# Mixing weights loaded right behind the taps' weight, five mixing and nine output places, another written-out order

## The reference

```python
w = softmax(weight, axis=-1)                       # 8 heads x 7 taps
out = einsum('hk,bskhg->bshg', w, x_unf)           # y: causal convolution of x
wq = y @ w_q; wk = y @ w_k                         # 192 -> 64
W_tok = (1 / sqrt(64)) * einsum('bsd,btd->bst', wq, wk)
mixed = einsum('bst,btd->bsd', W_tok, y)
return maximum(mixed, 0) @ w_out                   # 192 -> 192, float32
```

## Time and profile before

| what | us |
| --- | --- |
| median of three runs | 175.79 (175.0 to 176.97) |
| profiled execution, its own time | 176.94 |
| span of the profiled execution, first to last instruction | 175.2 |
| mean granted TensorE clock, share of full speed | 0.992 |

### The profile page before, as it was taken

How to read it: one execution, slowest core, us unless ns; L and a number is a source line. 1 busy time by engine, 2 the same in 40 slices (tenths; PEclk the granted TensorE clock), 3 DMA queues, 4 the chain that set the end, 5 groups by cost and what they waited for, 6 DMA issues and landing times.

```text
span 175.2 us, 6279 instructions
## 1 busy us (share of the span) xinstructions
PE 146.8 (84%) x2862; PEld 93.4 (53%) x2867; DVE 121.3 (69%) x187; ACT 113.7 (65%) x188; POOL 21.1 (12%) x23
## 2 busy tenths in 40 slices
PE   5987602198899899799999999999999998999980
PEld 1343302184357747465746665677657756675550
DVE  4514300546997799588868786899998859887660
ACT  2331401105993889667899878887988877797950
POOL 7982000200073005000000000000000000000000
PEclk9999999999999999999999999999999999999996
DMA  3999999999959999999920099972068998849796
GB/s 28 174 185 199 193 197 192 192 193 193 178 61 185 194 195 249 225 195 332 384 81 9 4 356 392 382 288 98 4 239 326 388 394 337 345 176 390 298 391 267
DMA packets 45388, 39.88 MB, mean 228 GB/s; under 512 B 35506, under 2 KB 37170, under 8 KB 45362
## 3 DMA queue, kind: packets, MB, share of 16 engines
q0 software_dynamic: 34080, 12.98, 62.5%
q1 hardware_dynamic: 11282, 26.51, 40.3%
HBM read 26.51 MB, written 25.95 MB: 299 GB/s over the span
## 4 chain that ended last, share of the span: by engine, by line
PE 60%; DMA 15%; DVE 9%; SPq 8%; issue 3%; ACT 1%; ACTq 0%; DVEq 0%; POOLq 0%
PE ps L723 12%; PE ps L915 11%; PE ps L898 11%; PE ps L590 10%; SPq L511 7%; DMA whi<-in_moe_w_k_dram 7%; PE ps L655 6%; DMA out_dram<-out_sb 5%; DVE y L622 4%; PE ps L818 4%; DMA xw<-in_x_dram 3%; PE ps L831 2%; DVE out_sb L933 2%; PE ps L278 1%; DVE rt L855 1%
## 5 line engine op out<-in xcount | busy, mean ns | idle before, releaser
L590 PE MATMUL ps<-xw,band 64*64 64x384 bf16 (+4 forms) x480 | 39.3, 332 | 5.8 <-issue 2.0
L723 PE MATMUL ps<-y 128*64 128x192 bf16 (+2 forms) x792 | 29.6, 232 | 12.1 <-ACT y L622 7.8
L933 ACT COPY out_sb<-ps 128x768 f32<-128x768 f32 (+1 forms) x47 | 34.6, 751 | 7.1 <-PE ps L915 6.5
L590 PE MATMUL ps<-xw,carry 64*64 64x384 bf16 (+2 forms) x160 | 38.1, 327 | 0.0
L854 ACT ACTIVATE rt<-ps 128x1024 bf16<-128x1024 f32 (+3 forms) x49 | 34.7, 732 | 4.8 <-PE ps L818 3.6
L622 ACT CAST y<-ps 128x792 bf16<-128x792 f32 (+3 forms) x46 | 30.6, 686 | 10.2 <-PE ps L590 9.8
L622 DVE CAST y<-ps 128x792 bf16<-128x792 f32 (+3 forms) x34 | 27.2, 816 | 13.1 <-PE ps L590 12.8
L723 PEld LDWEIGHTS ps<-y 128*64 128x64 bf16 x792 | 26.7, 118 | 15.5 <-ACT y L622 8.3
L637 DVE STREAM_TRANSPOSE yt<-y 128x768 uint32<-128x768 uint32 x32 | 30.1, 960 | 0.7 <-ACT y L622 0.5
L590 PEld LDWEIGHTS ps<-xw,band 64*64 64x64 bf16 x480 | 17.3, 114 | 21.5 <-PE ps L590 6.1
L855 DVE TENSOR_SCALAR rt<-ps 128x512 bf16<-128x512 f32 (+3 forms) x31 | 23.6, 769 | 7.2 <-PE ps L818 3.5
(11 more groups left out here) (105 smaller groups left out, 107.5 us busy)
## 6 DMA issues: line engine op xcount, KB each, us to landing
out_dram<-out_sb SPq DMA_DIRECT2D x28, 768.0 KB, 6.3
xw<-in_x_dram POOLq DMA_DIRECT2D x7, 816.0 KB, 23.0
xw<-in_x_dram POOLq DMA_DIRECT2D x7, 768.0 KB, 24.9
out_dram<-out_sb SPq DMA_DIRECT2D x8, 384.0 KB, 3.3
xw<-in_x_dram POOLq DMA_DIRECT2D x3, 384.0 KB, 9.0
out_dram<-out_sb SPq DMA_DIRECT2D x8, 96.0 KB, 3.2
xw<-in_x_dram POOLq DMA_DIRECT2D x1, 432.0 KB, 5.6
wq6f<-in_moe_w_q_dram SPq DMA_DIRECT2D x3, 64.0 KB
```

What stands on the lines that cost most here:

```text
L590: lambda p=p, a=a, w=w, back=back: e.matmul(at(op, p, a, z), w, XW[r : r + 64, s, a - back : z - back, g], start=start, stop=not start, sk ...
L723: mm = e.matmul(at[p : p + 64, o : o + z - r], Y[:, yb, c, r : r + 64], Y[:, yb, c, r:z], start=st, stop=end, skip_group_check=True,)
L933: return e.copy(dst, src) if op.letter == "A" else e.tensor_copy(dst, src)
```

## The change

The weight loads no longer wait for the taps' weight and for x; they have to stand behind the taps' weight in SP's order. `RT` has five places instead of four and `OUT` nine instead of ten. `PLAN` is another order of the same 929 operations, with other letters (engines and tilings) and banks in many places. In it SP's order is 0, 51, 49, 52, 50 (k, q, o, t) and then the stores. On ACT the order begins 16, 23, 56 (w_k), 32, 35, 30, 80, 74, 62 (w_out), 68, 71, 86, 101, 92, 61 (w_out), 59 (w_k), 54 (w_q, t), 107, 95, 110, 143, 128, 131, 55 (w_q, t), 113, 122, 116, 152, 53 (w_q). On DVE no cast of a weight other than w_k is left (57, 60, 58).

PE does the same products, of which some change their tiling. Between ACT and DVE some copies change places: ACT has 48 convolution casts (46 before), 42 output copies (47), 32 and 21 of the two relus (25 and 24), 15 scaled copies (8) and 6 of `gsb` (3).

```diff
 PLAN = """
-0S 4D 5D 2D 7D 1D 45G 3D 9D 13F 11G 46G 17D 8D 20D 12D 21D 47G 18D 14C0 15F 22D 16A 19D 23A 24D 48G 25D 26D 27D
-28C1 159G 31C2 29D 52S 160G 30A 34C3 36F 32D 35A 33A 78Q4 50S 37F6 261G 38F7 84Q0 69Q2 79Q 87Q6 85Q 80A 49S 88Q
-262G 86A 70Q 75Q4 89A 71D 63Q0 76Q 64Q 77D 96Q6 363G 97Q 93Q2 98A 51S 94Q 65A 105Q4 72Q6 95A 66Q0 106Q 364G 67Q
...
+0S 2D 6D 4D 5D 1D 51S 45G 13F 49S 11G 46G 12D 7D 9D 10D 14C0 15F 20D 17D 48G 3D 21D 52S 16A 18D 19D 22D 23A 47G
+24D 50S 25D 26D 27D 56A 159G 28C1 31C2 29D 160G 8D 34C3 36F 32A 35A 33D 30A 37C4 262G 63Q6 78Q0 261G 79Q 81Q2
+72Q4 80A 64Q 73Q 65D 82Q 66Q0 74A 83D 69Q6 363G 57D 70Q 67Q 84Q4 62A 75Q2 68A 85Q 71A 364G 86A 102Q0 99Q6 76Q
+96Q4 103Q 77D 97Q 104D 466G 90Q2 60D 98D 105Q0 91Q 100Q 93Q4 101A 92A 465G 108Q6 61A 87Q2 59A 106Q 94Q 54A 88Q
+107A 109Q 95A 89D 38C0 110A 137D 142C1 39F4 143A 123Q2 129Q6 126Q4 124Q 127Q 125D 130Q 117Q0 128A 118Q 131A
...
-    NX, NYT, NRT, NOUT = 5, 2, 4, 10
+    NX, NYT, NRT, NOUT = 5, 2, 5, 9
...
-            "S", emit, needs=[load_w, *load[0, 0]],
+            "S", emit, needs=[], after=[load_w],
```

More of the change, by code:

```diff
@@ L17 @@
 PLAN = """
-0S 4D 5D 2D 7D 1D 45G 3D 9D 13F 11G 46G 17D 8D 20D 12D 21D 47G 18D 14C0 15F 22D 16A 19D 23A 24D 48G 25D 26D 27D
-28C1 159G 31C2 29D 52S 160G 30A 34C3 36F 32D 35A 33A 78Q4 50S 37F6 261G 38F7 84Q0 69Q2 79Q 87Q6 85Q 80A 49S 88Q
-262G 86A 70Q 75Q4 89A 71D 63Q0 76Q 64Q 77D 96Q6 363G 97Q 93Q2 98A 51S 94Q 65A 105Q4 72Q6 95A 66Q0 106Q 364G 67Q
-107A 99Q2 68D 90Q4 81Q0 100Q 465G 91Q 82Q 101D 92D 83D 466G 120Q2 123Q4 73Q 117Q0 121Q 74A 118Q 61A 39F6 119D
-122A 124Q 129Q6 125A 126Q2 130Q 132Q0 127Q 131D 114Q4 133Q 115Q 135D 134A 102Q6 116A 108Q0 53A 111Q4 109Q 103Q
@@ new lines @@
+72Q4 80A 64Q 73Q 65D 82Q 66Q0 74A 83D 69Q6 363G 57D 70Q 67Q 84Q4 62A 75Q2 68A 85Q 71A 364G 86A 102Q0 99Q6 76Q
+96Q4 103Q 77D 97Q 104D 466G 90Q2 60D 98D 105Q0 91Q 100Q 93Q4 101A 92A 465G 108Q6 61A 87Q2 59A 106Q 94Q 54A 88Q
+107A 109Q 95A 89D 38C0 110A 137D 142C1 39F4 143A 123Q2 129Q6 126Q4 124Q 127Q 125D 130Q 117Q0 128A 118Q 131A
+111Q2 132Q4 119D 55A 112Q 133Q 120Q6 113A 114Q0 134D 115Q 121Q 58D 40C2 122A 568G 144C3 146C4 116A 147C 138D
+149C 135D 148C 151C 150C 136D 41F5 152A 53A 153F2 154D 155F6 139W04 156D 145D 157A 158A 164Q2 140A 141D 179Q6
@@ new lines @@
+165Q 180Q 181A 176Q0 166D 170Q4 177Q 171Q 178A 167Q6 172D 232Q2 168Q 161Q0 169A 234D 221Q4 162Q 223A 210Q2 163D
+231Q6 182Q4 233A 212D 183Q 173Q0 184D 174Q 235R2 175A 669G 209R6 236F 211D 275Q4 237A 567G 276Q 281Q0 186D 277A
+278Q6 266Q2 282Q 279Q 267Q 283A 196C4 268D 280A 254C5 198C 188D 201C 243Q0 220Q2 245A 187D 199C 256A 197C 222A
+200C 242R6 202D 224R0 185D 227R2 244A 203F5 225F 228F 204D 226A 189W64 229D 230S 238R0 191A 190D 246R2 239F 247F
+240A 272Q4 248D 192F6 205F7 193A 273Q 368Q0 206D 274A 371Q2 207D 369Q 208D 372Q 370D 263Q6 373A 269Q4 264Q 270Q
@@ new lines @@
+265A 216R0 271D 213R2 217F 214F 218D 380Q6 215A 284Q4 381Q 285Q 382A 365Q0 219S 286D 772G 386Q2 366Q 387Q 367A
+322R6 287D 298C4 670G 324A 311R0 290D 194C5 299C 313A 771G 300C 288D 388A 303C 249R6 289D 195A 333R0 253R2 250R
+335A 294C5 251D 301C 302C 255A 295A 252S 323Q0 304A 334Q6 377Q2 325A 336D 312Q4 378Q 314A 326R0 379D 344R6 327R
+346A 470Q4 328D 374Q2 471Q 375Q 472A 383Q6 376D 345Q0 384Q 347A 315R4 385D 305C2 316R 306A 257R3 337R0 317A 258R
+390D 318R6 338R 259A 319F 339A 260S 391D 291W42 241S 320A 389D 329R0 293A 292D 340R6 330R 341F 331A 307F2 342D
@@ new lines @@
+296C3 308A 351R4 348R0 309A 352F 297D 310D 396F6 349F 353A 397D 425Q2 350D 413R6 400C4 415A 427D 356C5 402C
+414Q0 446Q2 416D 447Q6 448A 404C 449D 405C 417R0 392D 435R2 424R6 437A 418R 426D 403C 401C 419A 488Q2 406D 358A
+482Q6 436Q0 489Q 473Q4 438A 483Q 490D 474Q 484A 428R0 475A 453R2 429R 355R6 454F 430D 357A 485Q4 455A 467Q6 486Q
+468Q 584Q0 487A 469D 476Q2 585Q 477Q 586A 450R4 407F6 451F 408A 478A 590Q0 452D 479Q6 591Q 480Q 359R2 592D 481A
+442R4 360R 409F3 443F 410A 491D 393W60 444A 411A 412A 361A 431R4 394A 395D 362S 420R2 432F 332S 421F 433A 343S
@@ new lines @@
+581Q6 422D 569Q0 354S 582Q 570Q 321S 548Q4 583A 502C2 550D 571A 506C 458C3 494D 515R6 460A 526R0 439R4 528A
+498F3 440F 493D 504C 517A 398C0 505C 499D 441D 503C 399A 507C 492D 445S 538Q6 508A 692Q0 516Q4 540A 693Q 518D
+677Q2 694A 527Q6 678Q 529D 537R4 679A 575Q0 539D 457R6 576Q 459A 572Q2 577A 587Q6 573Q 588Q 671Q4 574A 589D
+578Q0 672Q 579Q 673A 533R2 580D 530R6 534R 519R4 535D 531R 541R0 520R 532A 542F 521D 544R2 543A 509F6 545F 510D
+596D 522R4 546A 461R7 523F 462F 511F6 595D 495W02 512A 463A 524A 513D 514D 525S 560C7 604C6 497A 496D 434S 607C
@@ new lines @@
+456S 689Q4 562D 423S 686Q2 593D 629Q0 690Q 464S 687Q 631A 500C7 606C 691D 688A 609C 683Q0 501D 549Q2 594D 617Q4
+684Q 619A 608C 685D 605C 551A 600C7 618Q4 610A 601D 640Q0 782Q2 620A 642D 628Q6 783Q 630A 552R4 784D 555R0 553R
+556R 554A 621R6 650R2 557D 622F 652A 632R4 623D 558S 611F0 633F 612A 536S 791Q2 634A 651Q0 680Q6 653D 792Q 681Q
+793A 674Q4 682D 559R0 675Q 561A 676A 624R2 639R0 625R 641A 657R6 626D 635R4 658R 636R 659D 654R0 627S 646R2 637A
+655F 647F 656D 613F6 648A 643R4 563R7 644F 697D 614A 564F 597W02 615A 616A 645A 698D 706C6 599A 598D 662C4 707C
@@ new lines @@
+565A 788Q2 695D 664A 566S 752Q0 730Q4 649S 754A 789Q 732D 710C 547S 709C 790A 638S 660S 696D 720Q0 741Q4 722A
+753Q2 602C7 708C 743A 755D 711C 603D 742Q0 712A 773Q2 719Q4 744D 661Q6 774Q 721A 663D 748R0 775D 713F6 749F 714A
+731Q4 750A 779Q6 733D 794Q2 780Q 795Q 781A 785Q0 796D 776Q4 786Q 777Q 787A 723R6 778D 745R2 724R 726R0 746R 725D
+759R4 747A 727F 760F 797D 728A 699W62 799D 761A 729S 751S 665R0 737R4 701A 700D 715F1 738F 666F 739A 734R2 716D
+800D 756R6 717A 735R 718A 763R4 757R 736A 808C1 758D 667A 811C 740S 765A 762S 844Q2 833Q4 854Q6 846D 668S 813C
@@ new lines @@
+856A 809C 835D 764C0 832Q2 843Q4 834A 822Q6 845D 812C 810C 824A 821R2 814A 847R4 850R6 823A 815F1 848F 816D 851F
+766D 849D 825R0 852A 855Q2 798D 826R 857A 828R4 853S 767R6 829F 827D 817F7 830A 839R2 768F 840F 818D 831S 801W04
+841A 819A 820A 769A 836R2 770S 802A 803D 861R6 837F 862F 838A 858R0 863D 897R4 859F 899A 842S 42C2 860D 898Q6
+886Q2 900A 873Q4 888D 864S 910Q0 875A 901R6 912D 909R2 902R 911A 905R4 903D 885R0 906F 887A 702F2 904S 874Q6
+703D 907D 913R2 876A 893R0 914R 908S 894R 915A 881R6 895D 889R4 882R 916S 704C2 804C3 896S 705A 890R 805D 883A
@@ L62 @@
+866C0 891D 865Q1 806C3 867A 884S 868A 877R6 807A 917R1 869R0 892S 878F 918F 879A 43F3 919D 870F 922C4 871A 44F5
+880S 924A 921Q6 920S 923D 925R3 926F 927D 928S 872S
 """.split()
```

## The result

The changed kernel took 168.39 us in the median of four runs (167.53 to 169.37), the kernel before, beside it, 176.38: a ratio of 0.9555 (95% interval 0.9463 to 0.9647). The profiled execution took 169.37 us, 167.6 of them its span. So the span fell by 7.6 us, from 175.2.

A forecast was written before the change was run, and what follows sets the result against it. It took PE to set the pace (busy 84%) apart from one hole waiting for weights. 176.94 less 6.25 us for an earlier wq, zero behind it, gave 170.7 for the profiled execution, 169.5 in the median; range 163.5 to 174.8.

The forecast's parts named there:

- The hole: PE nearly idle from 20 to 34.5 us, busy 2.29 of 14.5, while DVE and ACT waited for weights.
- Landings: Weights asked for from 1.19 us at their old pace: w_k lands at 6.2, w_q 12.75, w_out 18.65, t 22.8.
- ACT waits for o, the convolution stops: ACT stands still until w_out lands at 18.65; PE stops in batch 0's convolution when its four bank pairs are full.
- hidden x: Batch 0's third piece of x lands between 15.1 and 22.8 us, hidden behind ACT's cast of t.
- From t to wq: From t at 22.8 through casts, third piece and Gram matmuls (27.15 to 32.85) to wq of batch 0 at 34.3.
- Behind wq: PE's 130 us after the start of wq: change taken as zero, bounds -4.9 to +2.9 us.
- Rival 1: Weights as slow as before from the new issue: last lands at 26.7, gain 2.35, time 173.4; chance 0.14.
- Rival 2: Weights come at once, ACT never waits: wq at 25.3, gain 15.2, time 160.6; chance 0.07.
- Rival 3: x of batch 1 becomes the limit: its convolution starts only 1 us sooner, time 174.8; chance 0.11.
- Rival 4: Slower by nine output places: copies wait for stores, four waits give 182.5; chance 0.12.
- no clock was lost in the hole: PE's granted clock, read as 1.00 in the hole and behind it, was taken to cost nothing there.

The follow-up runs named there:

- e1: Kernel before with only the wait of the weight loads removed, old order of work and old places: 168.75 us, ratio 0.9574.
- e2: Changed kernel with the old wait put back on the weight loads, new order and places kept: 175.85 us, ratio 0.9988.
- e8: Changed kernel with weights cut into transfers of 32, 64 or 128 rows and w_q's asked for last on SP: 158.09 us.
- e3: Changed kernel with ACT's casts of w_out and of w_q's second copy moved behind convolution casts of batch 0, loads untouched: 166.17 us.
- e10: Kernel before with the early ask and weights cut into transfers of 32, 64 or 128 rows, old order and places: 162.67 us.
- e4: Changed kernel with the same weight bytes cut into transfers of 32, 64 or 128 rows, nothing else changed: 164.00 us.
- e5: Kernel before with weights cut into transfers of 32, 64 or 128 rows, old wait kept: 166.31 us.

## Why the prediction was right, and where it was not

The forecast was 169.5 with a gain of 6.25 us of the span; measured were 168.39 and 7.6.

- *The hole ends when the last weight lands, and the early ask moves that.* Shown: e1 alone gives the gain, e2 without it gives none.
- *Landings.* k was put at 6.2, at most 8.3; it came at 8.83. Why so late is not shown; with the weights cut it came at 7.62 (e8). o (18.65) came at 20.37, t (22.8) at 24.55; from o to t it was 4.18, exactly the time read for t, and from k to o 11.54 where 12.45 were counted. So the pace taken from the old queue held to within a microsecond, and the start was too early by k's 2.6.
- *ACT waits for o, the convolution stops.* Right: 8.59 us, "near 7" forecast, and 0.53 for t. Two of the signs were missed by a little: the cast of w_out at 20.37 ("between 17 and 20") and wq at 36.03 ("between 32 and 36"). The third step of the chain, "hidden x", was only narrowly so: e3 shows x's third piece at 22.49, two us ahead of t.
- *From t to wq* I counted 11.5 us and 11.48 were measured, by errors that cancel, which is luck. The Gram matmuls began 6.03 us behind t where 4.35 were counted: I had let ACT's casts set this stretch and left out three fill-ups of 0.61 to 0.64 us on PE, and PE itself was busy 3.35 of the 3.50 us from 26.50 on, at a granted clock of 0.50. Then the Gram matmuls took 4.21 instead of 5.70, and the way from their end to wq 1.24 instead of 1.46.
- *Behind wq* I took zero of bounds from -4.9 to +2.9. Measured: -3.08. This is the term that was mis-sized, and that it made good the 1.73 that the start fell short is luck. The new order with its places does a part of it: it has 3.52 less behind wq with the old wait (e2 against before) and 2.90 less with early, cut weights (e8 against e10), but only 1.33 less than e1. For e1, in the old order with the old places, already has 1.75 less than the kernel before, in which PE stops for 1.22 us ahead of a convolution at 74.62; the profile names nothing that it waits for there, and e1 has no such stop. Each figure is of one execution, and those of the kernel before lie between 174.85 and 177.08 us, so differences below 1 us say little. Whether the order or the places do that part stays open: the order as written needs five places of `RT`, and ten of `OUT` beside them were not run.
- *Rival 1* (weights no faster) came about half: its last landing is 26.7, the forecast's 22.8, the measured 24.55. *Rival 2* (weights at once) did not come; e8 shows what it looks like once the transfers are cut, with wq at 25.31 where rival 2 has 25.3. *Rival 3* was half there: x's pieces were late, though not batch 1 but batch 0 was what had to wait (e1, e3). The rule of the Trainium skill that stood beside it ("DMA: Bandwidth & Descriptors", "Rules for kernel authors", an outermost dimension below 16 confines a transfer to that many engines) agrees with e4 and e5, which changed only that dimension and the number of transfers: w_k's wait of 12.10 us became 2.21. The two were not varied apart, and no view used here shows single engines. The 12.50 us that the prediction set beside the 2.9 of the taps' weight hold also the time behind the transfers issued earlier, so that comparison says less than e5 does. *Rival 4* (nine places): no output copy waited for a store in the profile after, where the kernel before had one.

## What to carry to other kernels

Before moving an ask earlier, look at how the transfer is cut: here the same bytes in transfers with an outermost dimension of 32 or more came sooner and delayed x less, and that one edit was worth more (e5, 166.31) than the early ask (e1, 168.75). Order a queue by the first use behind each transfer: moving w_q behind the two weights that are needed ahead of it was worth 3.7 us here. And an order that is written out fixes where an engine will wait: ACT stood still for 8.59 us ahead of a cast that nothing needed so early (e3). Read such a wait in the new profile before writing the next order.

## What the runs showed of the hardware that was not expected

The clock that the page prints can hide the pace. The Gram matmuls' pace in the kernel before (columns as above; 25 PE matmuls started in this microsecond), which prints 1.00:

```profile
36.00:37.00 1.00, 1.00 (x25) 1.00 (x23) 0.62 (x1) 0.00 (x0) 0.00 (x0) 1.00 1.60 192
```

and four stretches of the changed kernel:

```profile
6.00:8.00 2.00, 1.24 (x36) 0.82 (x36) 1.20 (x5) 0.00 (x0) 2.00 (x3) 1.00 1.41 173
8.00:10.00 2.00, 0.34 (x6) 0.16 (x4) 0.42 (x1) 1.12 (x4) 2.00 (x2) 0.81 1.44 184
32.00:33.00 1.00, 1.00 (x26) 1.00 (x23) 1.00 (x3) 0.00 (x0) 1.00 (x1) 0.50 1.55 185
33.00:34.00 1.00, 1.00 (x39) 1.00 (x35) 0.74 (x1) 0.00 (x0) 1.00 (x2) 0.93 1.62 191
```

In the changed kernel the granted clock begins to fall in the stretch in which PE is busy 0.34 of 2 us, is 0.50 (the 1.2 GHz level) later on, and rises by the stretch from 33 to 34, after PE had worked almost without a break from 26.5. At 0.50 it starts 26 of these matmuls in a microsecond, at 0.93, for the most part at the 2.4 GHz level, 39. The kernel before ran them at 25 with a printed 1.00, so at the lower level's pace. One fill-up (line 468, 512 columns) says the same: in the changed kernel it takes 0.61 us at a printed 0.50 (at 25.96) and 0.39 at a printed 1.00 (at 34.72), and in the kernel before 0.61 at a printed 1.00 (at 8.45). And the print differs between executions of one kernel: thirteen of the kernel before have a mean of 0.911 to 0.998, and their times do not follow it (175.40 us at 0.915, 174.96 at 0.993). What makes the print differ is not shown.

My sentence that no clock was lost in the hole rested on that print, and is wrong for the Gram stretch behind it: 5.70 us there, 4.21 in the changed kernel, and 3.06 in e8.
